# Attention score tiles over 64 rows of TensorE's array at a time, in place of sums stacked over 128 rows

## The reference, cut to what matters

```python
q_rot, k_rot = (rotate(q), rotate(k))
scale = 1.0 / np.sqrt(D)
scores = scale * np.matmul(q_rot, k_rot.transpose(0, 1, 3, 2))
scores = scores - np.max(scores, axis=-1, keepdims=True)
attn = np.exp(scores)
attn = attn / (np.sum(attn, axis=-1, keepdims=True) + 1e-09)
return np.matmul(attn, v).astype(np.float32)
```

## Time and profile before

| | |
|---|---|
| Median of three runs | 640.96 us |
| Span of the profiled execution | 639.07 us |
| Time around the span, median less span | 1.9 us |
| Attention, about | 0 to 291 us |
| TensorE busy | 621.5 us, 97% |
| VectorE busy | 509.4 us, 80% |
| ScalarE busy | 464.2 us, 73% |
| GpSimd busy | 341.0 us, 53% |
| TensorE instructions | 4724 matmuls, each with a weight load |

### The profile page before, as it was taken

The page is one execution under the profiler, slowest core; times in us unless marked ns, Lnnn a source line. Parts: engine busy times, 40 slices in busy tenths (PEclk is TensorE's granted clock), DMA queues, the critical chain, the costliest instruction groups (busy, mean ns, idle before and its releaser), DMA issues.

```text
span 639.1 us, 13808 instructions
## 1 busy us (share of the span) xinstructions
PE 621.5 (97%) x4724; PEld 604.7 (95%) x4724; DVE 509.4 (80%) x877; ACT 464.2 (73%) x1016; POOL 341.0 (53%) x316
## 2 busy tenths in 40 slices
PE   3899999999999999999999999999999999999997
PEld 3799999999999999999999999999999999999997
DVE  6899999999999999987385985569935499553895
ACT  3889999988889899986383664776556765567753
POOL 3999999998888887560900002860017800068200
PEclk9999999999999999999999999999999999999999
DMA  4767766767668774406001332000320002100002
GB/s 133 168 159 197 212 151 179 187 173 183 174 176 211 203 189 114 122 20 216 19 1 44 155 84 75 1 2 2 84 74 0 0 0 80 43 33 1 1 3 74
DMA packets 61898, 63.01 MB, mean 99 GB/s; under 512 B 18896, under 2 KB 46160, under 8 KB 61840
## 3 DMA queue, kind: packets, MB, share of 16 engines
q1 hardware_dynamic: 61392, 62.15, 35.7%
q10 hardware_dynamic: 448, 0.10, 0.1%
HBM read 31.46 MB, written 9.44 MB: 64 GB/s over the span
## 4 chain that ended last, share of the span: by engine, by line
PE 95%; SPq 1%; DVE 1%; DMA 1%; ACT 0%; issue 0%; ACTq 0%; DVEq 0%
PE slot L615 12%; PE rest L648 12%; PE rest L625 9%; PE slot L1344 8%; PE slot L1346 8%; PE slot L1345 8%; PE rest L1344 6%; PE rest L1346 6%; PE rest L1345 6%; PE rest L376 3%; PE rest L576 3%; PE rest L635 2%; PE slot L1376 2%; PE rest L1376 2%; PE rest L224 1%; PE rest L221 1%
## 5 line engine op out<-in xcount | busy, mean ns | idle before, releaser
L1335 POOL TENSOR_TENSOR w_ch_part<-w_ch_sums,w_ch_part 128x512 fp32r<-128x512 f32 x21 | 31.0, 1474 | 173.3 <-ACT w_ch_part L1588 173.3
L984 DVE TENSOR_REDUCE neg_max<-slot 128x1 f32<-128x576 f32 x142 | 106.7, 752 | 6.6 <-PE slot L615 2.2
L1652 ACT ACTIVATE pieces<-h 128x288 fp32r<-128x288 f32 x168 | 73.8, 444 | 49.8 <-PE slot L1346 25.3
L992 DVE TENSOR_TENSOR pt_lo<-rest,pt_hi 128x512 fp32r<-128x512 f32 x144 | 96.0, 677 | 1.9 <-ACT pt_hi L845 1.3
L648 PE MATMUL rest<-pt_hi,v 128*128 128x256 f32 (+1 forms) x320 | 89.3, 303 | 0.0
L845 ACT ACTIVATE pt_hi<-rest 128x512 fp32r<-128x512 f32 x144 | 84.1, 595 | 5.2 <-PE rest L625 4.3
L1743 DVE TENSOR_TENSOR pieces<-h,pieces 128x288 fp32r<-128x288 f32 x168 | 74.6, 454 | 9.4 <-ACT pieces L1652 8.9
L648 PE MATMUL rest<-pt_lo,v 128*128 128x256 f32 (+1 forms) x256 | 69.7, 295 | 0.0
L615 PE MATMUL slot<-key,q_hi 128*128 128x288 f32 x252 | 63.5, 333 | 2.2 <-ACT prob_a L838 1.0
L838 ACT ACTIVATE prob_a<-slot,neg_max 128x576 f32<-128x576 f32 x78 | 58.0, 743 | 10.1 <-DVE neg_max L984 10.0
L648 PEld LDWEIGHTS rest<-pt_hi,v 128*128 128x128 f32 x320 | 60.3, 188 | 0.1
(11 more groups left out here) (263 smaller groups left out, 2107.3 us busy)
## 6 DMA issues: line engine op xcount, KB each, us to landing
key<-t_hi_k SPq DMA_DIRECT2D x31, 144.0 KB, 2.3
key<-t_lo_k SPq DMA_DIRECT2D x31, 144.0 KB, 2.4
raw_qk<-in_q_dram SPq DMA_DIRECT2D x16, 256.0 KB, 2.8
raw_v<-in_v_dram SPq DMA_DIRECT2D x16, 256.0 KB, 3.3
x_scratch<-x_pair SPq DMA_DIRECT2D x16, 256.0 KB, 2.1
stage_or_x<-x_scratch SPq DMA_DIRECT2D x16, 256.0 KB, 4.3
q_hi<-t_hi_q SPq DMA_DIRECT2D x31, 128.0 KB, 2.4
q_cross<-t_hi_q SPq DMA_DIRECT2D x31, 128.0 KB, 2.4
```

The lines of the kernel that those rows point to most:

```text
L984: dve.tensor_reduce(neg_max[p % 2][:, i:i + 1], slot[g if 2 <= g < 4 else g % 2][:, :, 0:HALF], AX.XY, ALU.max, negate=True).then_inc(maxe ...
L992: dve.tensor_tensor(pt_lo[:, :, cols], rest[:, bank, :].rearrange("p (j n) -> p j n", j=G), f32(pt_hi[:, 0:G, cols]), ALU.subtract).then_i ...
L1652: act.activation(pieces[:, ring(m), 0, :], source[WEIGHTS[n]][:, ft, :], ACT.Copy).then_inc(piece_hi, 1)
```

## The change

For all tiles but the tail tiles and the first head's tiles of the first pair, the keys are cut in two halves of 288. One half is multiplied on the upper 64 rows of the array, the other on the lower 64 rows, each in three products (high by high, high by low, low by high), the upper and the lower in turn: six matmuls over 64 rows for four over 128. On the head's own rows operands are read from `t_hi` and `t_lo` directly; for the other rows, DMAs copy the queries' high and low part (`q_moved`) and half of the keys' (`k_moved`), four per head in place of five. The first head of the first pair keeps the stacked form in buffers of its own. The waits count four copies for five.

```diff
-    key = [sb(ctx, f"key{a}", [P, S], F32R) for a in range(2)]
-    q_cross = [sb(ctx, f"q_cross{a}", [P, MAIN], F32R) for a in range(2)]
-    q_hi = [sb(ctx, f"q_hi{a}", [P, MAIN], F32R) for a in range(2)]
+    first_key = sb(ctx, "first_key", [P, S], F32R)
+    k_moved = [sb(ctx, f"k_moved_{n}", [P, HALF], F32R) for n in ("hi", "lo")]
+    first_q_cross = sb(ctx, "first_q_cross", [P, MAIN], F32R)
+    first_q_hi = sb(ctx, "first_q_hi", [P, MAIN], F32R)
+    q_moved = [sb(ctx, f"q_moved_{n}", [P, MAIN], F32R) for n in ("hi", "lo")]
...
-    ASSEMBLED = 5 * 16
+    MOVED = 4 * 16
...
+        def move(n, a, p):
+
+            if no(p):
+                return
             top, low = slice(0, D), slice(D, P)
-            return (top, low) if a == 0 else (low, top)
-
-        def assemble_q(a, p):
-
-            if no(p):
-                return
-            i = p % 2
-            mine, other = halves(a)
-            sp.wait_ge(t_hi_done["q"], p + 1)
-            sp.dma_start(f32(q_hi[a][mine, :]), f32(t_hi["q"][i][mine, 0:MAIN])).then_inc(tiles_in[a], 16)
-            sp.dma_start(f32(q_cross[a][other, :]), f32(t_hi["q"][i][mine, 0:MAIN])).then_inc(tiles_in[a], 16)
-            sp.wait_ge(t_lo_done["q"], p + 1)
-            sp.dma_start(f32(q_cross[a][mine, :]), f32(t_lo["q"][i][mine, 0:MAIN])).then_inc(tiles_in[a], 16)
-
-        def assemble_k(a, p):
-
-            if no(p):
-                return
-            i = p % 2
-            mine, other = halves(a)
-            sp.wait_ge(t_hi_done["k"], p + 1)
-            sp.dma_start(f32(key[a][mine, :]), f32(t_hi["k"][i][mine, :])).then_inc(tiles_in[a], 16)
-            sp.wait_ge(t_lo_done["k"], p + 1)
-            sp.dma_start(f32(key[a][other, :]), f32(t_lo["k"][i][mine, :])).then_inc(tiles_in[a], 16)
+            here, there = ((top, low), (low, top))[a]
+            to = {"q": q_moved, "k": k_moved}[n]
+            cols = slice(0, MAIN) if n == "q" else (slice(HALF, S), slice(0, HALF))[a]
+            for part, (t, done) in enumerate(((t_hi, t_hi_done), (t_lo, t_lo_done))):
+                sp.wait_ge(done[n], p + 1)
+                sp.dma_start(f32(to[part][there, :]), f32(t[n][p % 2][here, cols])).then_inc(tiles_in[a], 16)
...
-        assemble_k(1, 0)
-        assemble_q(1, 0)
+        move("k", 1, 0)
+        move("q", 1, 0)
...
+            b = p % 2
             if i == G:
-                cols, b = slice(MAIN, W), p % 2
+                cols = slice(MAIN, W)
                 passes = ((t_hi["q"][b][:, cols], t_hi["k"][b]), (t_hi["q"][b][:, cols], t_lo["k"][b]),
                           (t_lo["q"][b][:, cols], t_hi["k"][b]))
+                passes = [[(queries, keys[:, f * HALF:(f + 1) * HALF]) for f in range(2)] for queries, keys in passes]
+            elif p == 0 and a == 0:
+                cols = slice(t * P, (t + 1) * P)
+                passes = [[(queries[:, cols], first_key[:, f * HALF:(f + 1) * HALF]) for f in range(2)]
+                          for queries in (first_q_hi, first_q_cross)]
             else:
-                cols = slice(t * P, (t + 1) * P)
-                passes = ((q_hi[a][:, cols], key[a]), (q_cross[a][:, cols], key[a]))
-            for n, (queries, keys) in enumerate(passes):
+                cols, mine, keys_here = slice(t * P, (t + 1) * P), slice(a * D, (a + 1) * D), slice(a * HALF, (a + 1) * HALF)
+                other = slice((1 - a) * D, (2 - a) * D)
+                passes = []
+                for qn, kn in ((0, 0), (0, 1), (1, 0)):
+                    here = ((t_hi, t_lo)[qn]["q"][b][mine, cols], (t_hi, t_lo)[kn]["k"][b][mine, keys_here])
+                    there = (q_moved[qn][other, cols], k_moved[kn][other, :])
+                    passes.append((here, there) if a == 0 else (there, here))
+            for n, halves in enumerate(passes):
                 if g == 0 and n == 1:
                     pe.wait_ge(first_hi, 4)
                     pe.wait_ge(first_lo, 2)
-                for f in range(2):
-                    mm = pe.matmul(s[:, f, 0:HALF], queries, keys[:, f * HALF:(f + 1) * HALF],
-                                   start=(n == 0), stop=(n == len(passes) - 1))
+                for f, (queries, keys) in enumerate(halves):
+                    mm = pe.matmul(s[:, f, 0:HALF], queries, keys, start=(n == 0), stop=(n == len(passes) - 1))
...
-        dve.memset(f32(q_hi[0][D:P, :]), 0.0).then_inc(zero_halves, 1)
-        dve.memset(f32(q_hi[1][0:D, :]), 0.0).then_inc(zero_halves, 1)
-        dve.wait_ge(zero_halves, 4)
+        dve.memset(f32(first_q_hi[D:P, :]), 0.0).then_inc(zero_halves, 1)
+        dve.wait_ge(zero_halves, 3)
```

More of the change, by code:

```diff
@@ L413, in load_next @@
             load(n, p)
-        def halves(a):
-            top, low = slice(0, D), slice(D, P)
-            return (top, low) if a == 0 else (low, top)
-        def assemble_q(a, p):
+        def move(n, a, p):
             if no(p):
                 return
-            i = p % 2
-            mine, other = halves(a)
-            sp.wait_ge(t_hi_done["q"], p + 1)
-            sp.dma_start(f32(q_hi[a][mine, :]), f32(t_hi["q"][i][mine, 0:MAIN])).then_inc(tiles_in[a], 16)
-            sp.dma_start(f32(q_cross[a][other, :]), f32(t_hi["q"][i][mine, 0:MAIN])).then_inc(tiles_in[a], 16)
-            sp.wait_ge(t_lo_done["q"], p + 1)
-            sp.dma_start(f32(q_cross[a][mine, :]), f32(t_lo["q"][i][mine, 0:MAIN])).then_inc(tiles_in[a], 16)
-        def assemble_k(a, p):
-            if no(p):
-                return
-            i = p % 2
-            mine, other = halves(a)
-            sp.wait_ge(t_hi_done["k"], p + 1)
-            sp.dma_start(f32(key[a][mine, :]), f32(t_hi["k"][i][mine, :])).then_inc(tiles_in[a], 16)
-            sp.wait_ge(t_lo_done["k"], p + 1)
-            sp.dma_start(f32(key[a][other, :]), f32(t_lo["k"][i][mine, :])).then_inc(tiles_in[a], 16)
+            top, low = slice(0, D), slice(D, P)
+            here, there = ((top, low), (low, top))[a]
[4 more added lines that the diff above has]
+                sp.dma_start(f32(to[part][there, :]), f32(t[n][p % 2][here, cols])).then_inc(tiles_in[a], 16)
         def store(p):
@@ L469, in sync @@
             sp.wait_ge(scores, p * TILES + G)
-            assemble_k(0, p + 1)
-            assemble_q(0, p + 1)
+            move("k", 0, p + 1)
+            move("q", 0, p + 1)
             load_next("k", p + 3)
@@ L475, in sync @@
             sp.wait_ge(scores, (p + 1) * TILES)
-            assemble_k(1, p + 1)
-            assemble_q(1, p + 1)
+            move("k", 1, p + 1)
+            move("q", 1, p + 1)
             if p == 0:
@@ L587, in score @@
             if t == 0 and g > 0:
-                pe.wait_ge(tiles_in[a], (p + a) * ASSEMBLED)
+                pe.wait_ge(tiles_in[a], (p + a) * MOVED)
             if g == 0:
-                pe.wait_ge(zero_halves, 4)
+                pe.wait_ge(zero_halves, 3)
                 pe.wait_ge(first_hi, 3)
@@ L823, in t_part_hi @@
                     if p - 2 + a > 0:
-                        act.wait_ge(tiles_in[a], (p - 2 + a) * ASSEMBLED)
+                        act.wait_ge(tiles_in[a], (p - 2 + a) * MOVED)
             act.activation(t_hi[n][p % 2][:], columns(bank, WIDE[n]), ACT.Copy,
@@ L876, in scalar @@
         act.wait_ge(t_hi_done["k"], 1)
-        act.activation(key[0][top, :], f32(t_hi["k"][0][top, :]), ACT.Copy).then_inc(first_hi, 1)
+        act.activation(first_key[top, :], f32(t_hi["k"][0][top, :]), ACT.Copy).then_inc(first_hi, 1)
         act.wait_ge(first_turned, 1)
@@ L880, in scalar @@
         act.wait_ge(first_hi, 2)
-        for to in (q_hi[0][top, EARLY_COLS[0]], q_cross[0][low, EARLY_COLS[0]]):
+        for to in (first_q_hi[top, EARLY_COLS[0]], first_q_cross[low, EARLY_COLS[0]]):
             act.activation(to, f32(q_first[top, EARLY_COLS[0]]), ACT.Copy).then_inc(first_hi, 1)
@@ L885, in scalar @@
         act.wait_ge(t_hi_done["q"], 1)
-        for to in (q_hi[0][top, EARLY_COLS[1]], q_cross[0][low, EARLY_COLS[1]]):
+        for to in (first_q_hi[top, EARLY_COLS[1]], first_q_cross[low, EARLY_COLS[1]]):
             act.activation(to, f32(q_first[top, EARLY_COLS[1]]), ACT.Copy).then_inc(first_hi, 1)
@@ L1020, in vector @@
         dve.memset(raw["q"][TAIL:P, 0, G, :], 0.0).then_inc(zero_halves, 1)
-        dve.memset(f32(q_hi[0][D:P, :]), 0.0).then_inc(zero_halves, 1)
-        dve.memset(f32(q_hi[1][0:D, :]), 0.0).then_inc(zero_halves, 1)
-        dve.wait_ge(zero_halves, 4)
+        dve.memset(f32(first_q_hi[D:P, :]), 0.0).then_inc(zero_halves, 1)
+        dve.wait_ge(zero_halves, 3)
         def key_lo():
             dve.wait_ge(t_hi_done["k"], 1)
-            dve.tensor_tensor(key[0][D:P, :], columns(0, S)[0:D, :], f32(t_hi["k"][0][0:D, :]), ALU.subtract).then_inc(first_lo, 1)
+            dve.tensor_tensor(first_key[D:P, :], columns(0, S)[0:D, :], f32(t_hi["k"][0][0:D, :]), ALU.subtract).then_inc(first_lo, 1)
         def q_lo(part):
             cols = EARLY_COLS[part]
```

(2 more changed lines are left out.)

## The result

The kernel after takes 662.18 us (661.95 to 662.36), the kernel before 640.93 us in the same job: a ratio of 1.033, 95% interval 1.0317 to 1.0342, so 21 us slower. The forecast was 660 us.

A forecast was written before the change was run, and what follows sets the result against it. TensorE was taken to bound the attention, VectorE close behind. 124 tiles x 0.19 us gave +23.4, or +16 if short waits go; +20 was taken on 640.96, so 661, given as 660; range 634 to 680 us.

The forecast's parts named there:

- The mechanism: In changed score tiles, weight loads bind, six in turn, and borders cost nothing: +0.19 us a tile; chance 0.34.
- A: Rival: in score tiles, pairs and their loads run side by side, so faster: 635 to 637 us; chance 0.33.
- B: Rival: score-tile pairs run side by side, but the array empties at borders: +0.19 us a tile, 658 to 665; chance 0.16.
- VectorE's fall to 89% of the attention: Sign named for loads binding: VectorE's share in the attention falls to about 90%, its waits naming the score line.
- Weight loads: Score tiles: six loads of 0.119 us in turn if one path serves both halves, 0.714 us, 0.19 more a tile.
- Borders: Array going from 128 rows to 64 and back around each changed tile, 248 times: taken as 0, upper bound 0.33 us a tile.
- The short waits: TensorE's waits in the attention, about 0.5 us an iteration, can go, lowering +23.4 us to +16; +20 taken.
- Copies, start and buffers: Fewer DMA copies per head, one memset gone at the start, t_hi and t_lo read longer: priced at nothing.
- The mixer: The stretch behind 291 us, untouched by the change: must keep its 348 us.

The follow-up runs named there:

- own_rows: Kernel after, with all six matmuls of a tile on the head's own 64 rows, so no two can run beside each other: 709.61 us, ratio 1.1071.
- borders_quarter: Kernel before, with q_hi by key over the head's 64 rows in only the first tile of each head, 31 tiles: 652.38 us, ratio 1.0177.
- borders_only: Kernel before, with q_hi by key over the head's 64 rows alone in 124 tiles, no pairs side by side: 686.47 us, ratio 1.0700.
- three_of_four: Kernel before, without q_hi by key for the second half of the keys in 124 tiles, three 128-row matmuls each: 635.74 us, ratio 0.9925.
- upper_then_lower: Kernel after, with a tile's three upper-row matmuls written before its three lower-row ones instead of in turn: 663.41 us, ratio 1.0348.
- values_128: all_64 with value products back on 128 rows; transposes and tail tiles stay at 64 rows: 664.30 us, ratio 1.0366 against the kernel before.
- all_64: Kernel after, with TensorE's other attention work also over 64 rows, lower halves left out, each transpose done as two: 842.45 us, ratio 1.3141.
- all_64_own: As all_64, with the six matmuls of a tile on the head's own 64 rows, so none runs beside another: 670.44 us, ratio 1.0450.

## Why the prediction was right, and where it was not

**The number and the sign** were right: 660 forecast, 662.18 measured, range 634 to 680. **The mechanism was not.** Two terms of the sum were wrong, one 0.32 us a tile too high and one 0.31 too low, and cancelled each other; that the forecast came within 2.2 us is luck. The signs that the prediction named say so too: starts came in near-coincident pairs 0.13 us apart, which it gave to A or B, and the ways in and out took 0.20 and 0.22 us, which is B. VectorE's fall to 89% of the attention, which it gave to the forecast, does not tell the two apart.

*Weight loads: "If one load path serves both halves of the array, a tile then takes 6 x 0.119 = 0.714 us".* This step failed. Both halves load at once, the pairs overlap wholly (0.394 a tile by `own_rows`), and the term is not +0.19 but -0.131 a tile. The load's own length came out as estimated: with nothing to hide behind, loads for the same rows are 0.11 us apart. (The kernel before has such a pair as well, the first two loads of a block of value products at 158.48 and 158.59, which is shorter than the 0.119 that the prediction calls the shortest; by 0.11 its term would have been 0.66 us a tile.) It is just not shared between upper and lower rows. No row of the kernel before could say so, as each load there fills all rows; "one after another" was read from a kernel that never asked for anything else.

*Borders: "I take 0 for the sum, since every kind of border that is seen costs nothing".* This step failed too. A way in and out costs 0.31 us in this kernel (0.37 where it leads to fp32r matmuls), at or above the upper bound of 0.33 that I kept for rival B. The borders that could be seen, between transposes and matmuls over the same 128 rows, were of another kind, and not evidence. The price has two parts in the trace, the array running empty (0.09 each way) and a first load that nothing hides (0.11, or 0.055 for transposes). The Trainium skill (TensorEngine Tiling (Array Packing), Key Properties) has the rule, "Mode switching requires drain", and the trace agrees, with those 0.09 us each way. By -0.131 and the 0.316 of `own_rows` the sum is 124 x 0.185 = 22.9 us, measured 21.2.

*Rival B*, at 0.16, is what happened, with 658 to 665 us as its time. It stood lower than the forecast for the reason just given. Its price was right in total only: it had 0.163 us of empty array each way, where the starts show 0.09, and no term for the loads that nothing hides, which make up the rest.

*The short waits* were to take in 3.4 of the 23.4 us. The starts give 0.20 + 0.16 for a way in and out, the iterations 0.315; the difference, 0.04 us a tile or some 5 us in all, is what they can have taken in, so this term was about right. They took it in everywhere alike, as the same slope in `borders_quarter` and `borders_only` shows.

*Rival A's price* held, 635 to 637 forecast and 635.74 measured with the borders' part taken away by other means. *Copies, start and buffers* were rightly priced at nothing: TensorE's one wait for the copies is 0.4 us in place of the 0.7 of the earlier trace rows, at the start, and no other wait of TensorE in the kernel after is for a DMA. *The mixer* kept its time.

No version among these beats the kernel before with the whole computation. By an estimate from these prices, which no run tested, one that did would need three or more neighbouring tiles between two borders (two save 0.262 us and pay 0.31), and in this order of work even two in a row brought 60 us of waits; the gain would be about the 5 us of `three_of_four` at most.

## What to carry to other kernels

Halving the rows of a matmul and running two beside each other worked fully in this kernel, loads included (fp32r, 128 columns of weights, 288 columns of output). But price a way from 128 rows to 64 and back at 0.31 to 0.37 us, two to three such matmuls: it pays only where the work between the two changes saves more than that, here by the estimate from three tiles in a row on. When a trace shows no example of a transition, its upper bound is as good a guess as zero, and two unknown terms of opposite sign should be argued together. Count how near the second engine is, too: here 1.05 us an iteration saved on TensorE were worth 0.34 (5.3 us over 15.5 iterations).

## What the runs showed that I had not expected

Matmuls on upper and on lower rows need not start in the order of the program: with three matmuls of the upper rows ahead in the program, the first of the lower rows started 0.01 us after the first of the upper (`upper_then_lower`), and in `values_128` a tile's matmul on the lower rows (151.90) overtook transposes on the upper (151.95). The Trainium skill (TensorE: Matmul & The Clock Gate, The mechanism) says that matmuls start and end in the order of the program; for starts on different rows this trace does not agree. The ends are modelled in the profile, so it can't speak of them. Whoever signals only on the last matmul of the program should see that it ends last; here the last pair's starts are 0.02 us apart.

And TensorE that is never idle can still be granted 1.2 GHz for 400 us (`all_64`, clock 0.50 from 60 to 460 us), when nearly all it does is over 64 rows. The same kernel with its value products over 128 rows, a change of one line, is `values_128` (on another chip), which had the upper level from 40 us on; and in `all_64` itself the clock was at 0.50 until 482 us and at 1.00 from 484, after the mixer's first matmuls over 128 rows at 481.06. That points at the work over 128 rows, but it can't be the whole of it: `all_64_own`, on the same chip as `all_64`, has no such work from 60 to 280 us either, and had the upper level there. What decides is open. The kernel after, with the same score tiles but the rest over 128 rows, had 2.4 GHz throughout.
